# The output stage of a three-layer kernel with another order of its block buffers, and two fewer tiles transposed by the matrix engine

## What is computed

```python
attn_out = _attn_ref(q, k, v)                  # 8 batches x 8 heads x 576 tokens x 64, keys and values pooled by 8
x = attn_out.transpose(0, 2, 1, 3).reshape(4608, 512)
x = _moe_ref(x, phi, w1, w2)                   # soft mixture: 8 experts with 4 slots each, result c @ slot_out
# _moe2_ref:
h = x @ w_in                                   # 4608 x 1024
e = np.exp(h - h.max(-1, keepdims=True))
sm = e / (e.sum(-1, keepdims=True) + 1e-09)
solu = h * sm
mu, var = solu.mean(-1), solu.var(-1)          # per token
ln = (solu - mu) / np.sqrt(var + 1e-06) * g_ln
return ln @ w_out                              # 4608 x 512
```

## Time and profile before

| | us |
|---|---|
| three runs | 472.50, 472.83, 475.33 |
| median | 472.83 |
| profiled execution, its own time | 472.24 |
| its span, first to last instruction | 470.4 |
| PE busy | 443.2 |
| DVE, ACT, POOL busy | 319.2, 254.0, 254.0 |
| granted TensorE clock, mean | 0.977 of full |

### The profile page before, as it was taken

The page is one execution under the profiler, slowest core; times in us unless marked ns, Lnnn a source line. Parts: engine busy times, 40 slices in busy tenths (PEclk is TensorE's granted clock), DMA queues, the critical chain, the costliest instruction groups (busy, mean ns, idle before and its releaser), DMA issues.

```text
span 470.4 us, 9944 instructions
## 1 busy us (share of the span) xinstructions
PE 443.2 (94%) x3498; PEld 348.2 (74%) x3498; DVE 319.2 (68%) x534; ACT 254.0 (54%) x550; POOL 254.0 (54%) x346
## 2 busy tenths in 40 slices
PE   5799999999999998999759999999999999999996
PEld 5677888888888874444338888888788888888875
DVE  7777677777768773645457997777677777777311
ACT  2474857667585753215238755555555555555310
POOL 0597886787888230102004236666666666666540
PEclk9898999999999999899888999999999999999999
DMA  8979898897989547999700146666666666666652
GB/s 267 295 233 296 272 309 222 316 302 257 337 196 307 198 160 263 346 369 397 304 0 1 45 69 136 126 135 130 135 133 135 135 134 135 136 132 136 135 120 45
DMA packets 125342, 91.70 MB, mean 195 GB/s; under 512 B 104824, under 2 KB 104832, under 8 KB 123264
## 3 DMA queue, kind: packets, MB, share of 16 engines
q1 hardware_dynamic: 125312, 91.32, 70.2%
HBM read 66.13 MB, written 9.44 MB: 161 GB/s over the span
## 4 chain that ended last, share of the span: by engine, by line
PE 41%; SPq 35%; DVE 8%; DMA 6%; issue 4%; ACT 4%; POOL 1%; DVEq 0%; ACTq 0%
SPq L448 32%; PE banks L1130 7%; DMA wslot<-in_moe_w 4%; PE banks L1182 4%; PE banks L1118 3%; SPq L437 3%; PE banks L1198 3%; PE banks L1162 3%; PE banks L1234 3%; PE banks L1349 2%; PE banks L1369 2%; PE banks L1206 2%; PE banks L1465 2%; PE banks L1467 2%; PE banks L1466 2%
## 5 line engine op out<-in xcount | busy, mean ns | idle before, releaser
L1465 PE MATMUL banks<-wo_hi,uh 128*128 128x512 f32 x288 | 112.8, 392 | 0.4 <-POOL ul L556 0.4
L1467 PE MATMUL banks<-wo_hi,ul 128*128 128x512 f32 x288 | 112.2, 389 | 0.0
L1466 PE MATMUL banks<-wo_lo,uh 128*128 128x512 f32 x288 | 112.1, 389 | 0.0
L556 POOL TENSOR_TENSOR ul<-u_col,uh 128x1024 fp32r<-128x1024 f32 x30 | 72.2, 2405 | 30.7 <-ACT uh L585 30.7
L482 POOL TENSOR_TENSOR attn<-attn,srec 128x576 f32<-128x576 f32 (+1 forms) x40 | 45.8, 1147 | 55.2 <-DVE srec L843 55.1
L776 ACT ACTIVATE sq<-u,usum 128x1024 f32<-128x1024 f32 x36 | 41.5, 1152 | 41.8 <-DVE u L1051 41.8
L1465 PEld LDWEIGHTS banks<-wo_hi,uh 128*128 128x128 f32 x288 | 54.2, 188 | 11.9 <-issue 0.8
L1467 PEld LDWEIGHTS banks<-wo_hi,ul 128*128 128x128 f32 x288 | 54.1, 188 | 11.3
L1466 PEld LDWEIGHTS banks<-wo_lo,uh 128*128 128x128 f32 x288 | 54.1, 188 | 11.1
L1041 DVE TENSOR_REDUCE nmax<-banks 128x1 f32<-128x1024 f32 x36 | 43.6, 1219 | 19.6 <-PE banks L1442 19.5
L1051 DVE SCALAR_TENSOR_TENSOR u<-banks,ex 128x1024 f32<-128x1024 f32 x36 | 43.7, 1221 | 15.3 <-ACT ex L769 15.0
(11 more groups left out here) (162 smaller groups left out, 735.1 us busy)
## 6 DMA issues: line engine op xcount, KB each, us to landing
wslot<-in_moe_w SPq DMA_DIRECT2D x14, 2048.0 KB, 9.8
u_col<-u_blk SPq DMA_DIRECT2D x240, 64.0 KB, 2.1
qb<-in_q SPq DMA_DIRECT2D x32, 256.0 KB, 6.4
out<-osb SPq DMA_DIRECT2D x32, 256.0 KB, 2.5
kraw<-in_k SPq DMA_DIRECT2D x8, 640.0 KB, 8.4
vraw<-in_v SPq DMA_DIRECT2D x8, 640.0 KB, 5.9
kraw<-in_k SPq DMA_DIRECT2D x8, 512.0 KB, 7.3
vraw<-in_v SPq DMA_DIRECT2D x8, 512.0 KB, 3.9
```

The lines of the kernel that those rows point to most:

```text
L556: pool.tensor_tensor(ul[par][:, :, :].rearrange("p c (q t) -> p (c q) t", q=4), v, uh[par][:, :, :].bitcast(F32).rearrange("p c (q t) -> p ...
L1465: pe.matmul(ps[4 + par], uh[par][:, c, :], wo_hi[:, c, :], start=(c == 0), stop=False)
L1466: pe.matmul(ps[4 + par], uh[par][:, c, :], wo_lo[:, c, :], start=False, stop=False)
L1467: last = pe.matmul(ps[4 + par], ul[par][:, c, :], wo_hi[:, c, :], start=False, stop=(c == FC - 1))
```

## The change

`LEAD` goes from 6 to 4, so tiles 4 and 5 are no longer transposed by PE: DVE makes their blocks and SP moves them, in a 16th shuffle that comes ahead of the others. The two block buffers are ordered (4, chunk, 2, 32) instead of (chunk, 4, 2, 32), so that what one DMA moves is one run of 2048 bytes in each of 32 partitions, where it was 8 runs of 256 bytes. The number of DMAs for a pair stays at 16, and their size at 64 KB. The reads and writes of the two buffers by DVE, ACT and POOL get access patterns with one more level. The rest of the diff follows from these two: in `moved`, the count of landings to wait for, and in `out_step`, the first shuffle.

```diff
-LEAD = 6
+LEAD = 4
...
-        u_blk = [bump(f"u_blk{i}", [P, FC, 4, 2, BLK]) for i in range(2)]
-        u_col = [bump(f"u_col{i}", [P, FC, 4, 2, BLK]) for i in range(2)]
+        u_blk = [bump(f"u_blk{i}", [P, 4, FC, 2, BLK]) for i in range(2)]
+        u_col = [bump(f"u_col{i}", [P, 4, FC, 2, BLK]) for i in range(2)]
...
         def moved(x, k):
 
-            return (x - k % 4) * 64 - (256 if k % 4 < 2 else 0)
+            return (x - k % 4) * 64
...
                 for q in range(4):
                     for j in range(4):
-                        sp.dma_start(u_col[slot][BLK * j:BLK * (j + 1), :, q, :, :], u_blk[slot][BLK * q:BLK * (q + 1), :, j, :, :]).then_inc(sem(f"u_col{slot}"), 16)
+                        sp.dma_start(u_col[slot][BLK * j:BLK * (j + 1), q, :, :, :].rearrange("p c t f -> p (c t f)"),
+                                     u_blk[slot][BLK * q:BLK * (q + 1), j, :, :, :].rearrange("p c t f -> p (c t f)")).then_inc(sem(f"u_col{slot}"), 16)
...
-                if k % 2 == 0 and not (isinstance(i, int) and (i < 2 or i + AHEAD >= OUT_TILES)):
+                if k % 2 == 0 and not (isinstance(i, int) and i + AHEAD >= OUT_TILES):
                     shuffle(i + 4, k + 4)
...
             def lo_col(x, k):
...
-                v = u_col[(k // 2) % 2][:, :, :, k % 2, :].rearrange("p c q t -> p (c q) t")
+                v = u_col[(k // 2) % 2][:, :, :, k % 2, :]
                 pool.wait_ge(sem("hi_col"), x + (1 - LEAD))
-                pool.tensor_tensor(ul[par][:, :, :].rearrange("p c (q t) -> p (c q) t", q=4), v,
-                                   uh[par][:, :, :].bitcast(F32).rearrange("p c (q t) -> p (c q) t", q=4), ALU.subtract).then_inc(sem("lo_col"), 1)
+                pool.tensor_tensor(ul[par][:, :, :].rearrange("p c (q t) -> p q c t", q=4), v,
+                                   uh[par][:, :, :].bitcast(F32).rearrange("p c (q t) -> p q c t", q=4), ALU.subtract).then_inc(sem("lo_col"), 1)
...
-                copy(uh[k % 2][:, :, :].rearrange("p c (q t) -> p (c q) t", q=4),
-                     u_col[slot][:, :, :, k % 2, :].rearrange("p c q t -> p (c q) t")).then_inc(sem("hi_col"), 1)
+                copy(uh[k % 2][:, :, :].rearrange("p c (q t) -> p q c t", q=4), u_col[slot][:, :, :, k % 2, :]).then_inc(sem("hi_col"), 1)
...
-                dve.transpose(u_blk[slot][:, :, :, k % 2, :].rearrange("p c q t -> p (c q) t"), u[k % URING][:, :].rearrange("p (b f) -> p b f", f=BLK)) \
+                dve.transpose(u_blk[slot][:, :, :, k % 2, :].rearrange("p j c t -> p c j t"), u[k % URING][:, :].rearrange("p (c j f) -> p c j f", j=4, f=BLK)) \
                     .then_inc(sem("u_blk"), 1)
```

## The result

| | before | changed |
|---|---|---|
| median of 20 runs, us | 472.33 | 475.74 |
| lowest to highest | 468.63 to 475.33 | 473.13 to 479.20 |
| ratio | | 1.0084 (1.0058 to 1.0110) |
| profiled execution | 472.24, span 470.4 | 473.32, span 471.5 |

The changed kernel is slower by 4.0 us (2.7 to 5.2) as the ratio has it, under 1%; the two medians alone differ by 3.4, inside the same interval. The forecast was 475.6, 3.3 above the profiled execution of before.

The account below looks back on a forecast made before the run. In the output stage PE was taken as full, with SP's shuffle queue at nearly the same pace. Shuffle +3.4, clock +1.5, waits -1.6 made +3.3 onto 472.24: 475.6 us, range 470.8 to 478.4.

Parts of the forecast that it names:

- The 16th shuffle decides: Ahead of out_t(4): SP's 16 new issues at 0.60 us each make PE wait for h_t(9)'s copy; +3.4 us.
- Rival A: SP's issue in the new form takes 0.43 us; out_t(4) +1.0, total 471.6; chance 0.22 with cases between it and the forecast.
- The clock: PE's idle time ahead of out_t(4) makes its clock fall once; +1.5 us, ends 0 and 3.4.
- rival B: SP stays the bound at 0.653 us an issue, the clock is low for two spells (3.4 us); 478.1 us, chance 0.18.
- The waits that go: After out_t(4): PE, 4.9 us late, no longer waits for SP's shuffles; -1.6 us.
- The saved transposes: Two tiles' transposes leave PE, 0.79 us each; the first leaves 0.2 to 0.3, hidden behind the shuffle; nothing in the sum.
- Access patterns: One more level in blocks, hi_col and lo_col on DVE, ACT and POOL; zero in the sum.

Follow-up runs that it names:

- DVE's order: Against the changed kernel, DVE's step 1 does u_mult of tiles 4 and 5 before both block transposes; 475.58 us, ratio 1.0076 to the kernel before.

## Why the prediction was right

Times from out_t(0), which takes the stage's own beginning out:

| step | forecast | measured |
|---|---|---|
| first issue of the new shuffle | 15.4 | 15.3 |
| its 16th issue | 25.2 | 25.6 |
| hi_col of tile 4 | 27.3 | 27.7 |
| copy to c4s done | 31.1 | 31.4 |
| out_t(4) | 31.7 | 32.5 |
| PE idle ahead of h_t(9) | 4.5 | 4.45 |

- *The 16th shuffle decides.* Right, in place, size and releaser. The price of an issue in the new form was taken as 0.60 and is 0.591; that is 0.2 less over the row, and the long first issue of my sum, 0.1 more, did not come; but one slow issue of 1.40, which the sum had not, cost 0.8, so the 16th issue came 0.4 late. About 0.2 of that was made good on the way to the copy. Rival A, an issue of 0.43, did not happen: the 256 issues have a median of 0.591 us and none took less than 0.512. The Trainium skill's table in "DMA: Bandwidth & Descriptors", section "Why a DMA increments its semaphore by 16 and not by 1", has 512 cycles for earlier generations; read as 0.43 us for an issue here, it does not agree with this trace. The landing is 2.0 instead of 2.1. The estimate in the prediction, from 3 cycles a packet in that page's section "Why small descriptors are slow (HBM only)", was 0.1 as well. But the same section says that transfers from SBUF to SBUF are free of that penalty, and no run here tells what made the difference.
- *The clock.* Right in kind. Expected +1.5; out_t(4) and h_t(9) together took 8.4 us instead of 5.9, +2.5. The clock was low for 6.9 us, about 2.0 of them under idle time, where the forecast had one fall of 3.4 and rival B two, nearly all of it under matmuls: between the two. That is the term that was mis-sized, by 1.0.
- *The waits that go.* Forecast -1.6, measured -1.5 (220.1 - 28.31 - 11.92 against the same of the changed kernel). The reason was right and not for the new form: LEAD 4 alone loses the waits too.
- *The saved transposes.* I had the first 0.79 go for 0.5 into a wait of h_t(8) for u of tile 6. The wait came one step earlier, at h_t(7) for u of tile 5, which now stands behind the block transpose of tile 4. I had moved the step behind the transposes and not the u_mult between them. It was 0.86 us, and the experiment with DVE's order shows it to be hidden behind the shuffle, as I had assumed for the wait of h_t(8).
- *Access patterns.* Zero, and zero in the trace: blocks 1.245, hi_col 1.060, lo_col 2.399, where they were 1.245, 1.058 and 2.405.
- *In rival A* I called 2 us of idle time too little to move the clock. In the kernel with four issues on ACT it fell behind 1.89 us. Had A come true, the step would have been wrong by 1.6.

The sum was +3.3 and the stage's +4.5: 1.0 more for the clock, and 0.2 for the slow issue less what was made good. The runs' 4.0 lies between, so a part of its nearness to 3.3 is luck.

## What to carry to other kernels

Before a job goes from a busy engine to a DMA queue, put its first use beside the queue's own pace: 16 issues in a row are 10 us before the last one even starts and 12.4 before it has landed, and here PE, with ACT's and POOL's part of the way taken off, wanted it landed about 8 us after the first issue. A prologue that looks like waste may be what covers the start of a queue; ask of each tile in it what would be late without it. And where two parts come in one change, measure each alone: the order gave 0.3 to 0.4% with LEAD 6, the shorter lead took 0.9%, and with both the loss was 0.8 to 1.1%, no smaller that the runs could tell, since the waits that the order takes away were gone already.

## What was not expected of the hardware

- The length of an issue on SP's queue hardly depends on the number of runs: 0.611 us with 256 runs of 256 bytes, 0.591 with 32 of 2 KB.
- An idle time of PE of 1.9 us in the midst of dense matmuls was followed by 3.4 us at 1.2 GHz, in one trace; filled with matmuls whose result nobody reads, in another, it was not followed by any.
- Single issues of 1.0 to 1.9 us come in every trace here, not always at the same place of the list: in the first shuffle of the changed kernel both times, in the second one in the kernel with DVE's order, whose list on SP is the same. They aren't scattered at random. Each trace has 16 KB packets that the page counts as "q8 instruction" (by the name, parts of the program itself), five of them from 240 us on. Of the 38 issues over 1.0 us in that part of the 13 traces, 36 start within 0.5 us of such a packet, and the other two within 0.2 us of an 8 KB one of "q14 instruction". In the changed kernel the issue starts at 268.50 and the packet at 268.56, in its second trace at 272.20 and 272.24; before, at 296.36 both. DMAs in flight at that time land late too, by 0.9 us in the changed kernel, by 1.8 in the kernel with 7 issues on ACT, there with the two stores beside them. In the trace of before one such packet comes at 270.80, when SP had nothing to issue, and costs nothing; in the changed kernel the new first shuffle stands there. That the one causes the other was not tested. The DMA queues of the changed kernel from 268.4 to 269.8 us:

```profile
q1 hardware_dynamic: 92, 0.13, 38.4%
q8 instruction: 1, 0.02, 5.1%
```

- Executions differ most ahead of the stage: out_t(0) starts anywhere from 246.9 to 255.7 us in these traces. In the latest of them, the kernel with 6 issues on ACT's queue, the clock is at 0.54 from 232 to 258, 23.9 us at 1.2 GHz, before the stage and in its first tile (a window, columns as in the earlier trace rows):

```profile
232.00:258.00 26.00, 20.08 (x96) 13.01 (x97) 14.04 (x21) 9.21 (x18) 4.24 (x16) 0.54 0.13 50
```

The three traces of the order alone say the same of one kernel: the stage begins at 248.7, 254.1 and 250.3 and then takes 219.1, 218.9 and 219.1. As far as these profiles show, the time ahead of the stage is where most of the runs' spread comes from, and it is the reason to compare stages from a common start.
